# Head 0's bucket bits in an attention and MLP kernel: float32 projections on a load of their own, and key bits written in place

## The reference

```
q_bits = (einsum('bhsd,dk->bhsk', q, proj) > 0)      # 6 bits per row
k_bits = (einsum('bhsd,dk->bhsk', k, proj) > 0)
q_bucket, k_bucket = sum(bits * 2 ** arange(6))
mask = q_bucket[:, :, :, None] == k_bucket[:, :, None, :]
scores = q @ k.T / sqrt(64);  scores = where(mask, scores, -1e9)
attn = softmax(scores);  x = attn @ v
x -> h = x @ w_in; g = s * relu(h)**2 + b; y = g @ w_out
y -> a = y @ w1; b = y @ w2; out = ((a * b) @ w3) @ w_out2
```

## Time and profile before

| what | us |
| --- | --- |
| median of three runs | 784.94 (783.82 to 785.97) |
| the profiled execution | 785.99 |
| its span, first to last instruction | 784.2 |
| PE busy | 756.1 (96% of the span) |
| DVE busy | 459.7 (59%) |
| ACT busy | 369.3 (47%) |
| POOL busy | 238.9 (30%) |
| DMA | 45.37 MB, mean 58 GB/s |

### The profile page before, as it was taken

One profiled execution on the slowest core, in us unless ns is written; L12 is line 12 of the kernel. 1 busy time (PEld: TensorE's weight loads), 2 busy tenths in 40 slices (PEclk: granted clock), 3 DMA queues, 4 the chain that ended last, 5 costly groups with the idle time before them and its releaser, 6 DMA issues.

```text
span 784.2 us, 11231 instructions
## 1 busy us (share of the span) xinstructions
PE 756.1 (96%) x3680; PEld 625.5 (80%) x3680; DVE 459.7 (59%) x809; ACT 369.3 (47%) x686; POOL 238.9 (30%) x150
## 2 busy tenths in 40 slices
PE   3999999999989899999999999999999999999998
PEld 2788888887778778888888888888887888888886
DVE  4899999999979821277565675666675201210220
ACT  2889998898879933353232232322342211211211
POOL 3347665575566663662021020210112000000000
PEclk9999999999989999999999999999999999999999
DMA  5353334333532223233010110101010000001001
GB/s 148 80 119 82 87 91 113 78 83 85 120 114 61 67 91 107 81 109 106 1 53 1 54 54 0 53 1 53 1 53 1 1 35 20 1 14 40 0 0 54
DMA packets 17680, 45.37 MB, mean 58 GB/s; under 512 B 4946, under 2 KB 6994, under 8 KB 17650
## 3 DMA queue, kind: packets, MB, share of 16 engines
q1 hardware_dynamic: 17650, 44.99, 20.7%
HBM read 37.75 MB, written 3.19 MB: 52 GB/s over the span
## 4 chain that ended last, share of the span: by engine, by line
PE 81%; DVE 7%; ACT 4%; issue 4%; DMA 2%; SPq 1%; POOL 0%; DVEq 0%; ACTq 0%
PE psum L986 54%; PE psum L1073 8%; PE psum L940 6%; PE psum L927 5%; PE psum L916 3%; DVE top L745 3%; PE psum L910 3%; ACT prob L524 2%; DVE pt_lo L759 1%; ACT pt_hi L540 1%; DVE x_lo L863 1%; PE psum L901 1%; DMA stage<-in_w_out 1%; DMA raw<-in_qk 1%; DVE qm L738 1%
## 5 line engine op out<-in xcount | busy, mean ns | idle before, releaser
L759 DVE TENSOR_TENSOR pt_lo<-psum,pt_hi 128x384 fp32r<-128x384 f32 x192 | 97.8, 549 | 12.7 <-ACT pt_hi L540 11.2
L524 ACT ACTIVATE prob<-psum,exp_at 128x768 f32<-128x768 f32 x96 | 96.3, 1003 | 11.2 <-DVE exp_at L752 11.1
L540 ACT ACTIVATE pt_hi<-psum 128x384 fp32r<-128x384 f32 x192 | 84.3, 494 | 20.3 <-PE psum L927 18.9
L745 DVE TENSOR_REDUCE top<-psum 128x1 f32<-128x768 f32 x96 | 90.9, 947 | 4.2 <-PE psum L916 4.0
L632 ACT ACTIVATE relu<-psum 128x512 f32<-128x512 f32 x48 | 28.6, 598 | 131.4 <-PE psum L986 131.4
L986 PE MATMUL psum<-x_hi,w_c 128*128 128x512 f32 (+1 forms) x288 | 88.7, 389 | 0.0
L986 PE MATMUL psum<-x_hi,w_b 128*128 128x512 f32 (+1 forms) x288 | 88.7, 389 | 0.0
L927 PE MATMUL psum<-ident,prob 128*128 128x128 f32 x576 | 83.8, 280 | 4.2 <-DVE pt_lo L759 3.9
L886 DVE TENSOR_TENSOR ab<-psum,a_sb 128x512 f32<-128x512 f32 x24 | 16.6, 691 | 117.8 <-ACT a_sb L682 117.8
L840 DVE SCALAR_TENSOR_TENSOR relu<-psum,relu 128x512 f32<-128x512 f32 x48 | 33.1, 689 | 84.8 <-ACT relu L632 79.8
L403 POOL TENSOR_TENSOR w_b<-stage,w_b 128x1024 fp32r<-128x1024 f32 x18 | 43.7, 2427 | 122.9 <-ACT w_b L551 122.2
(11 more groups left out here) (91 smaller groups left out, 1460.0 us busy)
## 6 DMA issues: line engine op xcount, KB each, us to landing
raw<-in_qk SPq DMA_DIRECT2D x30, 384.0 KB, 5.2
stage<-in_w_out SPq DMA_DIRECT2D x12, 512.0 KB, 3.3
stage<-in_w3t SPq DMA_DIRECT2D x8, 512.0 KB, 3.9
stage<-in_w_in SPq DMA_DIRECT2D x8, 512.0 KB, 3.2
stage<-in_w SPq DMA_DIRECT2D x8, 512.0 KB, 3.3
raw_v<-in_v SPq DMA_DIRECT2D x16, 192.0 KB, 2.7
qm<-both_hi SPq DMA_DIRECT2D x16, 192.0 KB, 2.7
r_sb<-r_rows SPq DMA_DIRECT2D x16, 192.0 KB, 5.4
```

The costliest lines, as they stand in the source:

```text
L524: act.activation(prob[:, t % 3], score[t % 2], ACT.Exp, bias=exp_at[:, t % 2, 1:2], scale=exp_at[:, t % 2, 0:1], accum_out=rsum[:, (t // 6 ...
L540: act.activation(pt_hi[:, u % 2, 3 * part:3 * part + 3, (t % 3) * P:(t % 3 + 1) * P], turned[part].rearrange("p (j q) -> p j q", j=3), ACT ...
L745: dve.tensor_reduce(top[:, t % 2, 1:2], score[t % 2], AX.X, ALU.max, negate=True).then_inc(top_done, 1)
L759: dve.tensor_tensor(pt_lo[at], turned[part].rearrange("p (j q) -> p j q", j=3), pt_hi[at].bitcast(F32), ALU.subtract).then_inc(pt_lo_done, 1)
```

## The change

It concerns head 0 alone, and the order in which a few instructions stand around it.

- ACT's own queue loads the projection `pj`, and then q and k of head 0 a third time: q to partitions 0 to 63 and k to 64 to 127 of `qk_first`, which is the first row of `x_raw`, a buffer that is free until the first output of head 0. Two transfers of 192 KB (64 x 768 float32). They stand before ACT's table load and first activation. SP's load of `pj` goes.
- DVE clears `pw_first` (128 x 128 float32, in `r_sb`, free for the same reason), and copies the float32 projection into it four times (query columns 64 and 76 from the lower partitions, key columns 96 and 102 from the upper).
- PE computes head 0's projections with two plain float32 matmuls of 128 x 384, one per half, into PSUM banks 4 and 5 (`turned`). They wait for `qk_first` and `pw_first`, not for any high or low part. The eight FR matmuls of head 0's two `dots` go.
- DVE writes head 0's bits with two instructions over both halves (18 x 768): the query's rows to partitions 64 to 81 of `qm`, the key's rows straight to partitions 64 to 81 of `km`. The two `bit_rows` and the copy of head 0's bits on SP go. Both stand ahead of `scale_q` of head 1.
- `k_lo(0)` moves from DVE to POOL, between `q_lo(0)` and `q_lo(1)`.
- On SP, the loads of head 2 and the copy of head 1's q stand ahead of the two small loads of `sb_col`.
- Heads 1 to 15 are computed as before.

```diff
--- before.py
+++ after.py
@@ -76,6 +76,8 @@
             pw = sb("pw", [P, 4, P], FR, a)
             pj_lo = sb("pj_lo", [P, BITS], FR, a)
             pj_hi = sb("pj_hi", [P, BITS], FR, a)
+            qk_first = x_raw[:, 0:SEQ]
+            pw_first = r_sb[:, 0:P]
             bit_from = sb("bit_from", [P, 1], F32, a)
             bit_weight = sb("bit_weight", [P, 1], F32, a)
             top = sb("top", [P, 2, 2], F32, a)
@@ -140,6 +142,7 @@
 
         qk_in = [sem("qk_in0"), sem("qk_in1")]
         first_q_in = sem("first_q_in")
+        qk_first_in = sem("qk_first_in")
         v_in = [sem("v_in0"), sem("v_in1")]
         proj_in = sem("proj_in")
         sb_in = sem("sb_in")
@@ -253,19 +256,16 @@
 
             for rows in HALVES:
                 sp.dma_start(raw[rows, 0, 0], qk[0, :, 0]).then_inc(first_q_in, 16)
-            sp.dma_start(pj[:, :],
-                         proj.unsqueeze(0).broadcast_to([2, HD, BITS])).then_inc(proj_in, 16)
             for rows in HALVES:
                 sp.dma_start(raw[rows, 0, 1], qk[0, :, 1]).then_inc(qk_in[0], 16)
             load_qk(1, 1)
             load_v(0, 0)
             load_v(1, 1)
+            copy_q_hi(0, 0)
+            load_qk(2, 0)
+            copy_q_hi(1, 1)
             sp.dma_start(sb_col[:, 0:1], s.partition_broadcast(P)).then_inc(sb_in, 16)
             sp.dma_start(sb_col[:, 1:2], b.partition_broadcast(P)).then_inc(sb_in, 16)
-            copy_q_hi(0, 0)
-            copy_bits(0, 0)
-            load_qk(2, 0)
-            copy_q_hi(1, 1)
             load_qk(3, 1)
 
             def pair(pr, last=False):
@@ -403,9 +403,12 @@
                 pool.tensor_tensor(lo, stage[:, slot, :], hi.bitcast(F32), ALU.subtract).then_inc(w_lo_done, 1)
 
 
-            for h in range(2):
-                q_lo(h, h)
-                pool.wait_ge(q_lo_done, h + 1)
+            q_lo(0, 0)
+            pool.wait_ge(q_lo_done, 1)
+            k_lo(0, 0)
+            pool.wait_ge(k_lo_done, 1)
+            q_lo(1, 1)
+            pool.wait_ge(q_lo_done, 2)
             v_lo(0, 0)
             pool.wait_ge(v_lo_done, 1)
 
@@ -550,6 +553,9 @@
                 act.wait_ge(staged[slot], 16 * count)
                 act.activation(hi, stage[:, slot, :], ACT.Copy).then_inc(w_hi_done, 1)
 
+            act.dma_start(pj[:, :], proj.unsqueeze(0).broadcast_to([2, HD, BITS])).then_inc(proj_in, 16)
+            for w, rows in enumerate(HALVES):
+                act.dma_start(qk_first[rows], qk[0, :, w]).then_inc(qk_first_in, 16)
             act.wait_ge(proj_in, 16)
             act.activation(pj_hi[:, :], pj[:, :], ACT.Copy).then_inc(pj_hi_done, 1)
             q_or_k_high(0, 0, 0, 0)
@@ -707,18 +713,22 @@
                                   ALU.subtract).then_inc(k_lo_done, 1)
 
 
+            dve.memset(pw_first, 0.0).then_inc(pw_clear, 1)
             dve.memset(pw[:, :, :].bitcast(F32), 0.0).then_inc(pw_clear, 1)
             dve.memset(bit_weight[64:96, :], 1.0).then_inc(pw_done, 1)
             dve.memset(top[:, :, 0:1], 1.0).then_inc(pw_done, 1)
             for k in range(2):
                 dve.memset(no_match[k], NO_MATCH).then_inc(pw_done, 1)
             dve.memset(rsum[:, :, :, 1:2], EPS).then_inc(pw_done, 1)
+            lower, upper = slice(0, HD), slice(HD, P)
+            dve.wait_ge(proj_in, 16)
+            dve.wait_ge(pw_clear, 2)
+            for rows, col in ((lower, 64), (lower, 76), (upper, 96), (upper, 102)):
+                dve.tensor_copy(pw_first[rows, col:col + BITS], pj[rows, :]).then_inc(pw_done, 1)
             scale_q(first_q_in, 0)
             dve.wait_ge(pj_hi_done, 1)
             dve.tensor_tensor(pj_lo[:, :], pj[:, :], pj_hi[:, :].bitcast(F32), ALU.subtract).then_inc(pj_lo_done, 1)
-            dve.wait_ge(pw_clear, 1)
             dve.wait_ge(pj_lo_done, 1)
-            lower, upper = slice(0, HD), slice(HD, P)
             for rows, w, col, part in ((slice(0, P), 0, 64, pj_hi), (slice(0, P), 0, 76, pj_hi),
                                        (slice(0, P), 1, 64, pj_lo), (slice(0, P), 1, 76, pj_lo),
                                        (lower, 2, 96, pj_hi), (lower, 2, 102, pj_hi),
@@ -781,10 +791,12 @@
                 dve.tensor_tensor(o_sum[rows, unit % 2], psum[rows, 6, 0:HALF], o_part[rows],
                                   ALU.add).then_inc(o_sum_done, 1)
 
-            k_lo(0)
+            dve.wait_ge(dots_done, 2)
+            for buf, rows, signal, count in ((qm, slice(64, 82), bits_done, 2), (km, slice(96, 114), bits_in[0], 16)):
+                dve.tensor_scalar(buf[64:82, 0].rearrange("r (c n) -> r c n", c=2), psum[rows, 4:6, 0:HALF],
+                                  bit_from[rows, :], bit_weight[rows, :], ALU.is_gt, ALU.mult).then_inc(signal, count)
             scale_q(qk_in[1], 1)
-            for c in range(2):
-                bit_rows(0, 0, c, 0)
+            dve.wait_ge(k_lo_done, 1)
             k_lo(1)
             for n in range(3):
                 top_of(n, n)
@@ -943,12 +955,14 @@
                     mm.then_inc(pv_done, 1)
 
             pe.wait_ge(rows_set, CONSTANTS)
-            pe.wait_ge(pw_done, 15)
+            pe.wait_ge(pw_done, 9)
+            pe.wait_ge(qk_first_in, 32)
+            for c in range(2):
+                pe.matmul(turned[c], pw_first, qk_first[:, c * HALF:(c + 1) * HALF],
+                          start=True, stop=True).then_inc(dots_done, 1)
+            pe.wait_ge(pw_done, 19)
             pe.wait_ge(q_lo_done, 1)
             pe.wait_ge(k_lo_done, 1)
-            dots(0, 0, 0)
-            pe.wait_ge(bits_done, 1)
-            dots(0, 0, 1)
             scores(0, 0, 0, 0)
             scores(1, 1, 0, 0)
             scores(2, 2, 0, 0)
```

## The result

The changed kernel takes 787.91 us (median of 9 runs, 786.01 to 790.31), the kernel before 785.12 us (median of 9, 783.82 to 786.77). The ratio is 1.0038, 95% interval 1.0022 to 1.0054: slower by about 3 us. The forecast was 783.0 with a range of 780.6 to 785.7. It was wrong in direction.

The account below looks back on a forecast made before the run. PE's back-to-back matmuls were taken to bound the kernel; only their start moves. The first row maximum at 16.2 instead of 18.23 takes 2.0 us off the median 784.94, forecast 783.0, range 780.6 to 785.7.

Parts of the forecast that it names:

- step 1: Transfers at the start: added 384 KB delay head 1's q and k from 10.67 to 12.0; `qk_first` is read at 6.2.
- the mark: Start of head 0's first row maximum, 18.23 in the kernel before, forecast at 16.2, 2.0 us earlier.
- Step 2: PE's two float32 matmuls for head 0: 1.28 us each plus 0.35 fill, so the dots end at 9.1.
- Step 3: Head 0's bits on DVE: 1.1 us for each of two instructions, ending at 11.3 instead of 17.08.
- Step 4: Head 1's preparation on DVE: `k_lo(1)` waits for POOL's `q_lo(1)` and ends at 16.2, where the first maximum starts.
- rivals A: Before the first maximum: POOL does not hold `k_lo(1)`, added bytes cost less; time 780.9 to 782.2, chance 27%.
- B's first clause: POOL's `v_lo` starts ahead of DVE's waiting `k_lo(1)`, so the first maximum starts at 17.3.
- rival C: On DVE, head 1's scaling waits behind the new bits for late float32 dots; at 14.5, 785.6 to 787.7; chance 8%.
- Rival D: PE's dots wait for the low parts, running 10.5 to 13.4; 1.6 us slower, no chance of its own.
- Behind the mark the lead stays: After the first maximum: the 2.0 us lead lasts, since every later load and buffer is released by an instruction moving with it.
- rival B: The lead is swallowed by POOL's `v_lo`, a late landing or PE's slower clock; time 784.0 to 785.9, chance 18%.
- Step 5: What is hidden at the start: moving `k_lo(0)` to POOL costs nothing; other copies and loads lie in waits.

Follow-up runs that it names:

- The kernel with a lead of 1.0: The changed kernel with head 0's third load queued on SP right behind q's first load, no longer on ACT: 785.74 us, ratio 0.9996.
- that with a lead of 0.8: The changed kernel with DVE's scaling of head 1's query ahead of the two instructions that write head 0's bits: 786.20 us, ratio 1.0008.
- the changed kernel's second profile: The changed kernel, unedited, timed again in a later session beside the kernel before: 787.38 us, ratio 1.0022.
- its filled version: The kernel before with 7 unread matmuls while PE waits for the copied bits and 3 before the first exponential: 782.54 us, ratio 0.9960.

## Why the prediction was wrong

**The step that failed is step 1's `qk_first` at 6.2** (bounds 5.2 and 6.5). It was read at 10.44, outside my bounds. Two assumptions made it. I gave each of ACT's issues 0.6 us, from SP's; the issue of the projection's load took 1.34, so the two loads were issued at 2.19 and 2.73, after SP had already issued the first of k. And I let them overtake what SP issued later. They did so only in part: the second one's landing took 7.58 us. From 4 to 8 us ACT's queue moved 156 of this load's 160 packets, and SP's, with k and a part of head 1, 187. The last four came after 8 us, and the load counts as landed only with them, at 10.31; why they came so late is not shown. The Trainium skill (DMA: Bandwidth & Descriptors, Queues, rings and completion order) says that the DMA engines take turns between the queues that have work. The trace agrees in kind, by these packet counts. On SP's queue, issued at nearly the same time (from 2.08), the same load was read at 7.31. So of the 4.2 us that my 6.2 was off, 1.1 stays even there, and 3.1 is the price of standing on the other queue, beside k and head 1, and not ahead of them.

**The same step's price of the bytes was too small.** I took 1.3 us on head 1's load, to 12.0. In the runs that wait for it, DVE starts on it at 12.98, 13.24 and 12.87, which is 2.2 to 2.6 after 10.69. The kernel before with the load alone gives 2.2 at the mark. My upper bound, 12.9, was the better value (in the changed kernel itself that load landed at 12.7), and no slack was left: the DMA engines are 0.99 busy there from 2.5 to 5 us.

**Step 2 was right.** Two float32 matmuls took 2.90, against 2.56 + 0.35 = 2.91: 1.28 each at 1.2 GHz, written as two records each. That is the cost of the four products, as the four passes of the Trainium skill (FP8 and Floating Point Precision, TensorE Precision Notes) have it, and not the two of the turns' row.

**Step 3 was right in size:** 1.07 and 1.09, against 1.1 each. It came 4.4 us late, at 15.68 instead of 11.3.

**Step 4 was right in mechanism.** `k_lo(1)` took 1.92 = 1.11 of waiting for POOL's `q_lo(1)` (17.98 to 19.09) and 0.81 of work, and DVE went ahead of `v_lo`; so rivals A and B's first clause fell. It was wrong in its start, since DVE reached head 1's scaling at 15.71 and not 12.0. My own rival C named that link and its threshold: dots that end after 9.8 move everything one for one, and from 11.8 the gain is gone. The dots ended at 13.36: 13.36 + 2.2 + 0.1 gives the scaling at 15.7, and the mark 1.7 behind. I gave this 8%, because I had looked for the danger in the matmuls' duration and held the landing for known within 6.5. Rival D's times (dots from 10.5 to 13.4, 1.6 us slower) were met almost to the tenth, but by luck: its cause, a wait for the low parts, was not there.

**"Behind the mark the lead stays" was wrong.** The kernel with a lead of 1.0 and that with a lead of 0.8 were no faster than before. Two things take it. One is PE's clock: the later it rises, the longer DVE and ACT wait for turns, and in the first profile this was 2.2 of the 3.2 us. I had that mechanism inside rival B and took it for part of a small case. PE idles 4.24 us ahead of tile 2, where it idled 1.14, but the length of that idle alone does not decide: the changed kernel's second profile has 4.64 and one slow group, the one with the scaling first 1.41 and two. That filling both waits takes the slow groups away, three profiles show; what else decides is open. The other is DVE's loop, 0.9 us by 213 us, which no step or rival of mine had (last section).

**Account of that profile's 3.2 us:** 1.7 at the mark, 2.2 more by the seventh maximum, 0.8 more by 202 us (last section), less 1.4 around 225 to 240, where both kernels lose the upper clock for a while after a stall; the lags at the maxima are 1.70, 3.93, 4.68 and 3.30.

**Step 5** (the move of `k_lo(0)` is free) held up to the mark. Behind it the move may cost 0.9 us; one profile speaks for that (last section).

## What to carry to other kernels

A load from a second queue is not an early load: where the engines are full, it takes its share of them and lands with its last packet, and what is urgent belongs at the head of the queue that feeds the chain. When an in-order engine gets a new wait, ask first which independent work of the next item stands behind it; here their order was worth some 2 us at the mark. And in a kernel that is bound by the matrix engine at the end but not at the start, throw-away matmuls in its waits can be worth as much as a shorter chain: 3 us in the kernel before, where a mark 2.9 us earlier gave 1.3 to 1.7. They are no sure gain: in the changed kernel 18 of them left the ratio at 1.0022.

## What the runs showed of the hardware that I had not expected

**The clock falls once more, and by how much differs from profile to profile.** The kernel before and its filled version both lose the upper clock near 222 us, behind a wait for weights. Windows of before, then of the filled one:

```profile
220.00:224.00 4.00, 2.70 (x13) 2.19 (x14) 3.85 (x8) 3.95 (x10) 3.84 (x3) 0.80 0.00 0
224.00:228.00 4.00, 4.00 (x17) 3.71 (x16) 2.78 (x5) 2.99 (x6) 2.79 (x2) 0.50 0.38 98
228.00:232.00 4.00, 4.00 (x25) 3.75 (x24) 2.83 (x9) 2.94 (x7) 1.82 (x1) 0.84 0.39 100
```

```profile
220.00:224.00 4.00, 4.00 (x19) 3.56 (x18) 3.40 (x7) 3.43 (x8) 3.76 (x4) 0.61 0.00 0
224.00:228.00 4.00, 4.00 (x29) 3.51 (x27) 3.64 (x9) 3.98 (x10) 3.17 (x2) 1.00 0.45 107
228.00:232.00 4.00, 4.00 (x26) 3.35 (x24) 3.90 (x9) 3.88 (x8) 0.98 (x2) 1.00 0.61 172
```

The filled kernel leads by 1.4 us before this place and by 3.2 behind it, in one execution each. Nothing was edited there. Over 212 to 236 us the mean granted clock is 0.86 in five of the twelve profiles (before among them), 0.93 in six and 1.00 in one, the kernel before with the third load. That one gains 2.6 us on the kernel before between the maxima at 213 and 231 us; the changed kernel gains 1.4 there in its first profile and 0.65 in its second. So this place is worth up to 2.6 us where the ends of two profiles are compared. What decides it is not shown; all nine runs of the filled kernel are faster than the fastest of the kernel before, and its profile explains 1.4 us of that.

**DVE loses 0.8 to 0.9 us in its loop over the pairs, without an edit there.** Waits of DVE (us in total, times, longest), before from 76 to 210 us and changed from 80 to 214 us:

```profile
DVE o_sum L781 <- issue: 1.1, 3, 0.4
```

```profile
DVE o_sum L791 <- issue: 1.9, 4, 0.5
```

The lag grows from 3.92 at 80 us to 4.68 at 202 and 4.81 at 213, in steps of 0.1 to 0.4, at DVE's first instruction of a round of the loop, ahead of which it stands for some 0.5 us waiting for nothing that the profile shows. All eight profiles of kernels with `k_lo(0)` on POOL have this growth, 0.8 to 0.9 from 84 to 213 us; it is what takes the rest of the lead of the kernel with the load on SP. The two kernels built on the kernel before have none. The one with `k_lo(0)` back on DVE has the first step of 0.4 and then falls back to no growth by 202 us. So the move of one instruction out of DVE's stream goes with the loss. Where a loop's instructions lie in an engine's stream may decide; no run here tests it.

**Head 0's q came later even without the third load.** With the projection's 3 KB on ACT's queue at the start, q was read by DVE at 5.52 and 5.71 in the two kernels without the third load, where it was read at 4.66 before. In these SP also issues k at 2.07 instead of 2.77, right behind q, and DVE's four copies end only at 5.2 or later. Which of the three it is, no run tells apart.
